# Attention scores of a chunk in two halves of 64 keys, in a token-mixer kernel

## The chip, the cores and the metric

The kernel runs on one core of a Trainium2 chip. The metric is the time of one execution on the device in microseconds (us), as a median of several executions.

## The reference

Three blocks follow one another: a gated linear attention, and two token and channel mixers. The change touches only the first. Cut to what matters, it is, for 4 batches, 8 heads, 768 tokens and 48 features a head:

```python
def _attn_ref(q, k, v, a_re, a_im):
    ...
    for t in range(S):
        new_re = ar * S_re - ai * S_im
        new_im = ar * S_im + ai * S_re
        kv = np.einsum('bhd,bhe->bhde', k[:, :, t], v[:, :, t])
        S_re, S_im = (new_re + kv, new_im)
        y[:, :, t] = np.einsum('bhd,bhde->bhe', q[:, :, t], S_re)
```

Each output row sees the keys and values of its own and of earlier tokens alone.

## The kernel before, in words

The four batches run one after the other. In each, the 768 tokens are cut into C = 6 chunks of P = 128. The real and imaginary parts of a head's 48 features stand together on 96 partitions (2 * HD), so that a token pair's decayed product is one product over 96 rows.

For a chunk c of a batch, TensorE works in the order written in `attention(b, c)`: `key_columns` (transposes of the chunk's keys), `scores(b, c, 0)` and `scores(b, c, 1)` (four heads each, into one PSUM bank each), `outputs` of the chunk before (transposes), `keys_values` (the chunk's contribution to the running state), `values` (scores times values, plus state times queries, into bank 3), and `turn_state` (transposes). In chunk 5 four `rank` products stand in the place of `keys_values`. A matmul on float32 operands is two passes in the trace, each with a weight load of its own.

The score bank holds, for a head, keys on the partitions and queries along the columns: 128 by 128. `mask_scores` on VectorE multiplies a bank of four heads by the triangle `tri` into `ST`, which `values` then takes as its moving operand. The even heads' results stand on partitions 0 to 47 of bank 3 and the odd heads' on 64 to 111 (`lo = 64 * (h % 2)`); `keys_values` is laid out in the same way.

VectorE's order in a batch is `mask_scores(b, c, 0)`, `mask_scores(b, c, 1)`, then `queries_keys(b, c + 2)` (one `scaled`, line 924, and two `turned`, line 937), then `next_state(b, c)`. The scaled queries and keys of chunk c + 2 go from SBUF to the tile `rows[c % 3]` by four DMAs in `to_rows` (lines 333 and 334), and `scores(b, c + 2)` waits for all four. The DMAs are issued from SyncE's one queue in program order; in a batch that order is `load_qk(b, c + 3)`, `load_v(b, c + 2)`, `to_rows(b, c + 2)`. `values` and `keys_values` wait for the semaphore `s_v_in` of `load_v` (line 317, tiles `v_in`), and `scaled` for that of `load_qk`.

At the start VectorE clears two PSUM banks (lines 1151 and 1152), GpSimd builds `tri` and the identity, ScalarE works on the first loads of a, and VectorE's first step of the real work is line 841. In batch 0 the conversion of the weights (ScalarE line 802, GpSimd line 506) runs between the chunks.

The rest of a batch, some 130 us of it, is made of the two mixers, with TensorE busy nearly throughout.

Of the kernel before, what the change touches and what calls it, by code (L numbers as in the profile page):

```python
# [8 lines left out]
ALU = mybir.AluOpType  # L9
ACT = mybir.ActivationFunctionType  # L10

P = 128
CONSTANTS = 6
# [13 lines left out]
        return b * (self.per_batch * self.unit) + (n + self.ahead) * self.unit  # L27


def token_mixer_program(nc, v, qk_rows, a_rows, U, V, w1, w2, w_tc, w_tok, out):  # L30
    B, S, D = v.shape
    HD = 48
    H = D // HD
    PAIRS = H // 2
    C = S // P
# [4 lines left out]
    N2 = HALF * P  # L40
    PIECES = C
    MID = P // 2
    G = D // P
    WIDE, FINE = 2 * HD // G, HD // G
    assert FINE * H == P and 2 * WIDE * H // 2 == 2 * P and C == 2 * G and G == 3
    assert N2 == D and H * HD == D and 3 * R <= P and F * P == 2 * C * P and F == 2 * C
    assert 2 * D == C * P

    with ExitStack() as ctx:
        def sb(name, shape, dt=F32):  # L50
            return ctx.enter_context(nc.sbuf_tensor(name, shape, dt))

        def sem(name, per_batch, unit=1, ahead=0):
            return Count(ctx.enter_context(nc.semaphore(name)), per_batch, unit, ahead)
# [11 lines left out]
        tc_raw = nc.alloc_sbuf_tensor_at("tc_raw", [P, 2 * KD, D], F32, offset=tc_at + 2 * KD * D * 4)  # L66
        U3 = sb("U3", [P, C, 3, R])
        V3 = sb("V3", [3 * R, S], F32R)
        tri = sb("tri", [P, P])
        ident = sb("ident", [P, P])  # L70
        half_pi = sb("half_pi", [P, 1])
        ln_eps = sb("ln_eps", [P, 1])
# [1 line left out]

        marks = sb("marks", [P, 2, G, C])
        minus_mid = sb("minus_mid", [P, G, C])
        gain = sb("gain", [P, G, C - 1])
        gain_rows = sb("gain_rows", [P, H, C - 1])
        carry = sb("carry", [P, G])

# [7 lines left out]
        stream = sb("stream", [P, 4 * 2 * S])  # L88
# [6 lines left out]
        angle = ((tA, tB), (tC, tD))  # L95
        v_in = (stream[:, 8 * D:9 * D], stream[:, 9 * D:10 * D], tD[:, :])
        KV = tA[:, :].rearrange("p (j d) -> p j d", j=PAIRS)
        scale = sb("scale", [P, 2, G, 2, P])
        qk_at = nc.sbuf_base
        qk = sb("qk", [P, 6 * D])  # L100
# [5 lines left out]
        ST = sb("ST", [P, H, P])  # L106
# [7 lines left out]
        rows = [at.rearrange("p (h j t) -> p h j t", h=H, j=2) for at in rows_at]  # L114
# [63 lines left out]
        score_bank = (bank[6], bank[7])  # L178
# [5 lines left out]
        def heads(ap, n=4):  # L184
            return ap.rearrange("p (h t) -> p h t", h=n)


        s_const = sem("s_const", 0)
        s_zero = sem("s_zero", 0)
# [9 lines left out]
        s_a_first = [sem(f"s_a_first{c}", 0, 16) for c in range(C)]  # L199
        s_a_in = [sem(f"s_a_in{i}", 2 if i + A_BUFS < C else 1, 16) for i in range(A_BUFS)]  # L200
        s_qk_in = [sem(f"s_qk_in{i}", C // 2, 16) for i in range(2)]
        s_v_in = [sem(f"s_v_in{i}", C // 3, 16) for i in range(3)]
        s_rows_in = [sem(f"s_rows_in{i}", C // 3, 64) for i in range(3)]
        s_gain_in = sem("s_gain_in", 1, 64)
        s_sq = sem("s_sq", C)
# [93 lines left out]
        def _(sp):  # L299
# [13 lines left out]
            def load_v(b, c):  # L313

                if c >= 3:
                    sp.wait_ge(s_yt.sem, s_yt.at(b, c - 2))
                sp.dma_start(v_in[c % 3], v[b, c * P:(c + 1) * P, :]).then_inc(s_v_in[c % 3].sem, 16)

            def to_rows(b, c):

                if c >= 3:
                    sp.wait_ge(s_yt.sem, s_yt.at(b, c - 2))
                elif b and c == 2:
                    sp.wait_ge(s_ch.sem, s_ch.at(b - 1, 2 * KD))
                elif b and c == 1:
                    sp.wait_ge(s_mix.sem, s_mix.at(b - 1, 2 * C))
                elif b:
                    sp.wait_ge(s_mix.sem, s_mix.at(b - 1, 2 * C - 2))
                to = rows[c % 3]
                for r in range(2 if b or c else 1):  # L330
                    sp.wait_ge(s_Q.sem, s_Q.at(b, c) + r + 1)
                    wide, fine = row(r)
                    sp.dma_start(to[wide, :, :, :], QKz[c % 2][:, r, 0:2, :, :]).then_inc(s_rows_in[c % 3].sem, 16)  # L333
                    sp.dma_start(to[fine, :, :, :], QKz[c % 2][:, r, 2, :, :]).then_inc(s_rows_in[c % 3].sem, 16)
# [42 lines left out]
            def batch(b, last):  # L377
# [36 lines left out]
                if not last:  # L414
                    sp.wait_ge(s_mix.sem, s_mix.at(b, 2 * C - 3))
                    load_qk(b_next, 0)
                    load_qk(b_next, 1)
                    gains_to_rows(b_next)
                    to_rows(b_next, 0)
                    load_qk(b_next, 2)  # L420
                    sp.wait_ge(s_mix.sem, s_mix.at(b, 2 * C))
                    load_v(b_next, 0)
                    load_v(b_next, 1)
# [139 lines left out]
        def _(act):  # L563
# [92 lines left out]
            def attention(b, c):  # L656
# [6 lines left out]
                if c + 1 < C:  # L663
# [3 lines left out]
                    elif b:  # L667
                        act.wait_ge(s_stored[2].sem, s_stored[2].at(b, 0))
                    a.activation(KV[0:112, :, :], bank[4][0:112, 0:D].rearrange("p (j d) -> p j d", j=PAIRS), ACT.Copy)\
                        .then_inc(s_kv_sb.sem, 1)  # L670
# [165 lines left out]
        def _(dve):  # L836
            d = nc.vector
# [15 lines left out]
            def log_decay(b, c):  # L853
# [11 lines left out]
                if b and i == 0:  # L865
                    dve.wait_ge(s_exp.sem, s_exp.at(b - 1, (half + 1) * G))
                d.tensor_copy(marks[:, :, i, half * G:(half + 1) * G],
                              ln_m2.rearrange("p (t e m) -> p e t m", e=2, m=MID)[:, :, :, MID - 1]).then_inc(s_marks.sem, 1)
                if i == G - 1:
# [75 lines left out]
            def mask_scores(b, c, i):  # L945
                dve.wait_ge(s_score.sem, s_score.at(b, 2 * c + i + 1))
                if c >= 1 and i == 0:
                    dve.wait_ge(s_yt.sem, s_yt.at(b, c))
                elif c == 0 and b:
                    for n in range(2 - i):  # L950
                        dve.wait_ge(s_stored[n].sem, s_stored[n].at(b, 0))
                elif c == 0:
                    dve.wait_ge(s_v3.sem, 2)
                d.tensor_tensor(ST[:, 4 * i:4 * i + 4, :], heads(score_bank[i][:, :]),  # L954
                                tri[:, :].unsqueeze(1).broadcast_to([P, 4, P]), ALU.mult)\
                    .then_inc(s_score_sb.sem, 1)

            def next_state(b, c):
# [190 lines left out]


            d.memset(bank[3][:, :], 0.0).then_inc(s_zero.sem, 1)
            d.memset(bank[4][:, :], 0.0).then_inc(s_zero.sem, 1)

            for c in range(C + 2):
# [22 lines left out]
        def _(pe):  # L1177
            t = nc.tensor

            def mm(o, lhsT, rhs, start=True, stop=True, turned=False):  # L1180
                return t.matmul(o, lhsT, rhs, start=start, stop=stop, is_transpose=turned)  # L1181

            def key_columns(b, c):
                if c >= 1:
                    pe.wait_ge(s_kn.sem, s_kn.at(b, c))
                elif b:
                    pe.wait_ge(s_out.sem, s_out.at(b - 1, 2))
                for r in range(2):
                    pe.wait_ge(s_Q.sem, s_Q.at(b, c) + r + 1)
                    for i in range(G):  # L1190
                        ins = t.transpose(bank[r][:, i * P:(i + 1) * P], QKz[c % 2][:, r, i, 1, :], ident[:, :])  # L1191
                    ins.then_inc(s_ktr.sem, 1)

            def scores(b, c, i):
                pe.wait_ge(s_rows_in[c % 3].sem, s_rows_in[c % 3].at(b, c // 3 + 1))
                if c >= 1:
                    pe.wait_ge(s_score_sb.sem, s_score_sb.at(b, 2 * c - 1 + i))
                for h in range(4):
                    ins = mm(heads(score_bank[i][:, :])[:, h, :], rows[c % 3][0:2 * HD, 4 * i + h, 1, :],
                             rows[c % 3][0:2 * HD, 4 * i + h, 0, :])  # L1200
                ins.then_inc(s_score.sem, 1)

            def keys_values(b, c):
# [12 lines left out]
            def turn_state(b, c):  # L1216
# [3 lines left out]
                for j in range(PAIRS):  # L1220
                    ins = t.transpose(heads(bank[2][0:2 * HD, :])[:, j, 0:112], KV[0:112, j, :], ident[0:112, 0:112])  # L1221
                ins.then_inc(s_kv_t.sem, 1)

            def values(b, c):
                pe.wait_ge(s_v_in[c % 3].sem, s_v_in[c % 3].at(b, c // 3 + 1))
                if c >= 1:
                    pe.wait_ge(s_yt_sb.sem, s_yt_sb.at(b, c))
                    pe.wait_ge(s_state.sem, s_state.at(b, c))
                elif b:
                    pe.wait_ge(s_out.sem, s_out.at(b, 0))  # L1230
                for h in range(H):
                    if h % 4 == 0:
                        pe.wait_ge(s_score_sb.sem, s_score_sb.at(b, 2 * c + h // 4 + 1))
                    lo = 64 * (h % 2)
                    o = heads(bank[3][lo:lo + HD, :])[:, h // 2, :]
                    ins = mm(o, v_in[c % 3][:, h * HD:(h + 1) * HD], ST[:, h, :], stop=c == 0)
                    if c >= 1:
                        ins = mm(o, state[0:2 * HD, h, :], rows[c % 3][0:2 * HD, h, 0, :], start=False)
                ins.then_inc(s_yt.sem, 1)
# [207 lines left out]
                        key_columns(b_next, 0)  # L1447

            pe.wait_ge(s_const.sem, CONSTANTS)
            pe.wait_ge(s_zero.sem, 2)  # L1450
            key_columns(0, 0)
            for b in range(B - 1):
                batch(b, False)
# [50 lines left out]
```

## Time and profile before

| | |
|---|---|
| median of 3 executions | 779.67 us (779.47 to 780.95) |
| profiled execution | 780.54 us, of which the span is 778.8 us |
| TensorE busy (matmul) | 710.3 us, 91% |
| VectorE busy | 503.9 us, 65% |
| ScalarE busy | 417.3 us, 54% |
| mean granted TensorE clock | 0.991 |

The profile shows one execution. The span is from its first to its last instruction. PE is TensorE's matmuls, PEld its weight loads, DVE is VectorE, ACT ScalarE, POOL GpSimd and SPq the queue of SyncE, which issues DMAs. Starts in the timeline and in the chain of waits are in us from the span's start. A name such as `bank<-region` is output from input.

### The profile page before, as it was taken

The numbers are of one execution on the slowest core, as the hardware profiler recorded it, in microseconds if no ns is written. First come the engines' busy times: TensorE is split into PE (matmuls) and PEld (weight loads), VectorE is DVE, ScalarE is ACT, GpSimd is POOL, SyncE is SP. The second block draws the span as 40 slices with busy tenths as digits, with TensorE's granted clock in tenths as the row PEclk, the third lists the DMA queues.
The fourth block names the chain that finished last, engine by engine and source line by source line (L and its number), as shares of the span: only waits on it lengthen the run. The fifth ranks groups of instructions, "written<-read, shape, count | busy, mean of one in ns | idle before, by whom it ended". The sixth has DMA issues, their size and how long they took to land.

```text
span 778.8 us, 13125 instructions
## 1 busy us (share of the span) xinstructions
PE 710.3 (91%) x4944; PEld 683.4 (88%) x4944; DVE 503.9 (65%) x918; ACT 417.3 (54%) x913; POOL 220.8 (28%) x175
## 2 busy tenths in 40 slices
PE   0028999999999999999999999999999999999998
PEld 0027879999999979999999979999999879999998
DVE  6978858699458758597458747597448832224634
ACT  8875757665464636673464637674463621223531
POOL 0003582433430053222530053223440000113350
PEclk9998999999999999999999999999999999999999
DMA  9645540010246850010136950010136840000121
GB/s 325 201 110 144 146 176 5 1 42 1 61 120 192 218 203 21 1 42 0 61 104 193 235 203 21 0 42 1 42 103 183 227 144 37 1 1 1 42 61 61
DMA packets 42734, 73.45 MB, mean 94 GB/s; under 512 B 8784, under 2 KB 23376, under 8 KB 42672
## 3 DMA queue, kind: packets, MB, share of 16 engines
q1 hardware_dynamic: 42384, 72.23, 31.6%
q8 instruction: 39, 0.64, 0.4%
q10 hardware_dynamic: 288, 0.39, 0.2%
q14 instruction: 23, 0.19, 0.1%
HBM read 48.96 MB, written 4.72 MB: 69 GB/s over the span
## 4 chain that ended last, share of the span: by engine, by line
PE 83%; DVE 7%; ACT 4%; DMA 3%; issue 2%; SPq 1%; DVEq 0%; ACTq 0%
PE bank L1181 80%; DMA region<-qk 2%; PE bank L1351 1%; DVE stream L924 1%; PE bank L1262 1%; PE bank L1191 1%; PE bank L1221 1%; DMA region<-stream 1%; DVE logr L862 1%; DVE ST L954 1%; DVE qk L937 1%; DVE phasor L913 0%; DVE phasor L904 0%; SPq L333 0%; ACT scale L626 0%
## 5 line engine op out<-in xcount | busy, mean ns | idle before, releaser
L1181 PE MATMUL bank<-uT,w_sb 128*128 128x384 f32 x864 | 167.8, 342 | 0.0
L1181 PE MATMUL bank<-hT,w_sb 128*128 128x384 f32 x864 | 165.0, 337 | 0.0
L1181 PE MATMUL bank<-tok,z 128*128 128x384 f32 x864 | 158.7, 337 | 0.6 <-issue 0.2
L1181 PEld LDWEIGHTS bank<-uT,w_sb 128*128 128x128 f32 x864 | 153.1, 192 | 1.5 <-ACT uT L691 1.2
L1181 PEld LDWEIGHTS bank<-hT,w_sb 128*128 128x128 f32 x864 | 151.2, 188 | 0.3 <-DVE hT L1083 0.3
L1181 PEld LDWEIGHTS bank<-tok,z 128*128 128x128 f32 x864 | 149.3, 188 | 1.8 <-POOL tok L511 1.8
L1083 DVE SCALAR_TENSOR_TENSOR hT<-bank,hT 128x384 fp32r<-128x384 f32 x96 | 52.8, 550 | 72.0 <-ACT hT L683 71.7
L683 ACT ACTIVATE hT<-bank 128x384 fp32r<-128x384 f32 x96 | 46.5, 484 | 83.3 <-PE bank L1181 83.1
L511 POOL TENSOR_TENSOR tok<-tok_low,tok 128x768 fp32r<-128x768 f32 x20 | 38.1, 1907 | 86.8 <-ACT tok L713 86.8
L1191 PE MATMUL bank<-ident,stream 128*128 128x128 f32 x72 | 11.3, 297 | 48.6 <-DVE stream L937 48.6
L519 POOL TENSOR_TENSOR x_sb<-uT 128x384 f32<-128x384 f32 x24 | 25.1, 1074 | 102.2 <-DVE uT L1077 69.2
L1191 PEld LDWEIGHTS bank<-ident,stream 128*128 128x128 f32 x72 | 9.1, 154 | 49.0 <-issue 48.6
L506 POOL TENSOR_TENSOR w_sb<-w_raw,w_sb 128x768 fp32r<-128x768 f32 x12 | 23.8, 1999 | 75.9 <-ACT w_sb L802 75.9
L525 POOL TENSOR_TENSOR xs<-x_sb,xs 128x384 fp32r<-128x384 f32 x24 | 27.7, 1170 | 54.5 <-ACT xs L700 54.5
L488 POOL TENSOR_TENSOR logr<-stream 128x384 f32<-128x384 f32 x18 | 14.9, 826 | 95.8 <-DMA stream<-in_a 95.7
L1181 PE MATMUL bank<-tc_sb,xs 128*128 128x384 f32 x216 | 41.4, 336 | 0.0
L493 POOL TENSOR_TENSOR phasor<-stream,phasor 128x384 f32<-128x384 f32 x18 | 19.1, 1062 | 74.4 <-ACT phasor L599 74.4
L954 DVE TENSOR_TENSOR ST<-bank,tri 128x512 f32<-128x512 f32 x48 | 32.4, 686 | 11.2 <-PE bank L1181 11.0
L1181 PE MATMUL bank<-region 96*128 96x128 f32 x256 | 33.4, 286 | 6.6 <-DMA region<-stream 4.8
L1181 PE MATMUL bank<-xs,tc_sb 128*128 128x384 f32 x216 | 38.9, 338 | 0.0
L1181 PEld LDWEIGHTS bank<-region 96*128 96x128 f32 x256 | 31.7, 201 | 7.7 <-DMA region<-stream 5.2
L1181 PEld LDWEIGHTS bank<-tc_sb,xs 128*128 128x128 f32 x216 | 37.9, 188 | 0.0
(147 smaller groups left out, 1310.7 us busy)
## 6 DMA issues: line engine op xcount, KB each, us to landing
stream<-in_qk SPq DMA_DIRECT2D x24, 384.0 KB, 3.8
tok_low<-in_w_tok SPq DMA_DIRECT2D x20, 384.0 KB, 3.5
stream<-in_a SPq DMA_DIRECT2D x19, 384.0 KB, 4.4
scale<-in_w_tok SPq DMA_DIRECT2D x16, 384.0 KB, 4.2
w_raw<-in_w SPq DMA_DIRECT2D x12, 384.0 KB, 7.6
region<-qk SPq DMA_DIRECT2D x16, 256.0 KB, 3.6
region<-stream SPq DMA_DIRECT2D x15, 256.0 KB, 3.1
stream<-in_v SPq DMA_DIRECT2D x16, 192.0 KB, 4.9
```

Of the source, the lines that this page charges most:

```text
L488: ins = g.tensor_tensor(to, part, part, ALU.mult)
L493: g.tensor_tensor(phasor[:, c, 1, :], a_part(b, c, 1), phasor[:, c, 1, :], ALU.mult)\
L506: g.tensor_tensor(part[1], raw, part[0].bitcast(F32), ALU.subtract).then_inc(s_split.sem, 1)
L511: g.tensor_tensor(tok[:, m % 4, 1, :], tok_raw(m)[1], tok[:, m % 4, 0, :].bitcast(F32), ALU.subtract)\
L519: g.tensor_tensor(x_sb[:, n, :], uT[:, 0, kd, :].bitcast(F32), uT[:, 1, kd, :].bitcast(F32), ALU.add)\
L525: g.tensor_tensor(xs[0][:, 1, n % KD, :], x_sb[:, n, :], xs[0][:, 0, n % KD, :].bitcast(F32), ALU.subtract)\
L683: a.activation(hT[:, n % 3, 0, :], hidden_bank[n % 3][:, 0:N2], ACT.Relu).then_inc(s_hid_hi.sem, 1)
L862: ins = d.tensor_tensor_scan(ln_m2[:, cols], ln_m2[:, cols], cor[:, cols], 0.0, ALU.add, ALU.subtract)
L954: d.tensor_tensor(ST[:, 4 * i:4 * i + 4, :], heads(score_bank[i][:, :]), tri[:, :].unsqueeze(1).broadcast_to([P, 4, P]), ALU.mult)\
L1083: d.scalar_tensor_tensor(hT[:, n % 3, 1, :], hidden_bank[n % 3][:, 0:N2], 0.0, hT[:, n % 3, 0, :].bitcast(F32), ALU.max, ALU.subtract)\
L1181: return t.matmul(o, lhsT, rhs, start=start, stop=stop, is_transpose=turned)
L1191: ins = t.transpose(bank[r][:, i * P:(i + 1) * P], QKz[c % 2][:, r, i, 1, :], ident[:, :])
```

## The change

The scores of a head are no longer one matmul of 128 keys by 128 queries but two: the first 64 keys with all 128 queries, and the last 64 keys with the last 64 queries. What is left uncomputed is the quarter that the triangle sets to zero. For an even head the first keys stand on partitions 0 to 63 of the bank; for an odd head the halves are exchanged. `mask_scores` therefore multiplies by `both_tri`, the triangle and the triangle with its halves exchanged. The values of the odd heads are needed in the same exchanged order of tokens, and come from DRAM a second time, as an array prepared on the host, by a load of [128, 192] for each chunk. The score banks are cleared once at the start.

```diff
+        both_tri = sb("both_tri", [P, 2, P])
+        tri = both_tri[:, 0, :]
+        v_turned_sb = sb("v_turned_sb", [P, 2, PAIRS * HD])
...
                 sp.dma_start(v_in[c % 3], v[b, c * P:(c + 1) * P, :]).then_inc(s_v_in[c % 3].sem, 16)
+                sp.dma_start(v_odd[c % 3], v_turned[b, c * P:(c + 1) * P, :]).then_inc(s_v_in[c % 3].sem, 16)
...
-                d.tensor_tensor(ST[:, 4 * i:4 * i + 4, :], heads(score_bank[i][:, :]),
-                                tri[:, :].unsqueeze(1).broadcast_to([P, 4, P]), ALU.mult)\
+                d.tensor_tensor(ST[:, 4 * i:4 * i + 4, :].rearrange("p (j e) t -> p j e t", e=2),
+                                score_bank[i][:, :].rearrange("p (j e t) -> p j e t", e=2, t=P),
+                                both_tri[:, :, :].unsqueeze(1).broadcast_to([P, 2, 2, P]), ALU.mult)\
...
             d.memset(bank[3][:, :], 0.0).then_inc(s_zero.sem, 1)
+            for i in range(2):
+                d.memset(score_bank[i][:, :], 0.0).then_inc(s_zero.sem, 1)
+            dve.wait_ge(s_const.sem, CONSTANTS)
+            d.tensor_copy(both_tri[0:MID, 1, :], tri[MID:P, :])
+            d.tensor_copy(both_tri[MID:P, 1, :], tri[0:MID, :]).then_inc(s_tri.sem, 1)
+            dve.wait_ge(s_tri.sem, 1)
             d.memset(bank[4][:, :], 0.0).then_inc(s_zero.sem, 1)
...
-                for h in range(4):
-                    ins = mm(heads(score_bank[i][:, :])[:, h, :], rows[c % 3][0:2 * HD, 4 * i + h, 1, :],
-                             rows[c % 3][0:2 * HD, 4 * i + h, 0, :])
+                for pair in range(2):
+                    for late in range(2):
+                        for odd in range(2):
+                            h, lo, t0 = 2 * pair + odd, MID * (odd ^ late), MID * late
+                            ins = mm(heads(score_bank[i][lo:lo + MID, :])[:, h, t0:P],
+                                     rows[c % 3][0:2 * HD, 4 * i + h, 1, t0:t0 + MID],
+                                     rows[c % 3][0:2 * HD, 4 * i + h, 0, t0:P])
...
-                    ins = mm(o, v_in[c % 3][:, h * HD:(h + 1) * HD], ST[:, h, :], stop=c == 0)
+                    of = v_odd[c % 3][:, h // 2 * HD:(h // 2 + 1) * HD] if h % 2 else v_in[c % 3][:, h * HD:(h + 1) * HD]
+                    ins = mm(o, of, ST[:, h, :], stop=c == 0)
```

## Rows read from the trace of the kernel before

**Rows 1.** The page: busy time of the engines, and the shares of the chain that ended last.

```profile
PE 710.3 (91%) x4944; PEld 683.4 (88%) x4944; DVE 503.9 (65%) x918; ACT 417.3 (54%) x913; POOL 220.8 (28%) x175
...
PE 83%; DVE 7%; ACT 4%; DMA 3%; issue 2%; SPq 1%; DVEq 0%; ACTq 0%
```

**Rows 2.** Groups by form, TensorE: busy us, mean ns of one, idle before (scores, values, keys_values).

```profile
L1181 PE MATMUL bank<-region 96*128 96x128 f32 x256 | 33.4, 286 | 6.6 <-DMA region<-stream 4.8 <-DMA region<-qk 1.7
L1181 PE MATMUL bank<-ST,stream 128*48 128x128 f32 x256 | 26.5, 292 | 3.9 <-DVE ST L954 3.8
...
L1181 PE MATMUL bank<-qk,stream 128*48 128x96 f32 x256 | 14.5, 258 | 0.3
```

**Rows 3.** Timeline of TensorE, batch 1, chunk 1 and the start of chunk 2: start, duration.

```profile
250.52 0.87 PE L1181 MATMUL bank<-qk,stream 128*48 128x96 f32 x16
251.22 0.42 PE L1181 MATMUL bank<-ST,stream 128*48 128x128 f32 x4
...
252.75 0.42 PE L1181 MATMUL bank<-stream,state 96*48 96x128 f32 x4
253.11 0.59 PE L1221 MATMUL bank<-ident,tA 112*96 112x112 f32 x4
253.53 0.82 PE L1191 MATMUL bank<-ident,stream 128*128 128x128 f32 x6
254.19 1.95 PE L1181 MATMUL bank<-region 96*128 96x128 f32 x16
```

**Rows 4.** The chain that ended last, batch 1, chunks 0 to 3: start, duration, what.

```profile
246.22 0.96 DVE stream L924
...
251.27 0.96 DVE stream L924
...
255.19 5.42 DMA region<-qk
260.62 0.04 issue
260.66 2.05 PE bank L1181 x16
```

**Rows 5.** The same chain in batches 2 and 3, the last DMA before chunk 3.

```profile
431.97 5.21 DMA region<-qk
...
610.02 6.40 DMA region<-qk
```

**Rows 6.** Timeline of batch 1: a load of values, and two waits for a DMA.

```profile
251.93 0.43 SPq L317 DMA_DIRECT2D stream<-in_v  x1
...
257.37 0.96 DVE L924 TENSOR_TENSOR stream<-stream,scale 128x768 f32<-128x768 f32 x1 [0.50 <-DMA stream<-in_qk]
...
260.66 1.60 PE L1181 MATMUL bank<-region 96*128 96x128 f32 x12 [0.36 <-DMA region<-qk]
```

**Rows 7.** DMA issues of the page: count, size, median us from issue to landing.

```profile
stream<-in_qk SPq DMA_DIRECT2D x24, 384.0 KB, 3.8
...
stream<-in_v SPq DMA_DIRECT2D x16, 192.0 KB, 4.9
```

**Rows 8.** Stretch of 4 us in batch 1: busy time of each engine, clock, DMA share, GB/s.

```profile
256.00:260.00 4.00, 4.00 (x63) 3.67 (x62) 3.29 (x4) 2.46 (x7) 0.00 (x0) 1.00 1.09 277
```

**Rows 9.** Timeline of batch 0, chunks 0 and 1.

```profile
55.06 3.78 PE L1181 MATMUL bank<-region 96*128 96x128 f32 x16 [4.77 <-DMA region<-stream]
...
58.77 1.52 PE L1181 MATMUL bank<-qk,stream 128*48 128x96 f32 x16
...
61.91 0.59 PE L1221 MATMUL bank<-ident,tA 112*96 112x112 f32 x4
...
69.92 0.67 PE L1181 MATMUL bank<-ST,stream 128*48 128x128 f32 x4 [3.63 <-DVE ST L954]
```

**Rows 10.** A stretch of batch 0: busy time of each engine, granted clock (0.51), DMA.

```profile
68.60:72.00 3.40, 2.08 (x20) 2.09 (x22) 3.35 (x5) 2.31 (x3) 0.00 (x0) 0.51 0.02 5
```

**Rows 11.** Timeline of VectorE at the start.

```profile
1.52 0.48 DVE L1152 MEMSET bank<- 128x512 f32 x1
...
4.96 0.56 DVE L841 SCALAR_TENSOR_TENSOR logr<-logr,phasor 128x384 f32<-128x384 f32 x1 [2.95 <-ACT phasor L583]
```

More of the change, by code:

```diff
@@ L27, in at, with token_mixer_program @@
         return b * (self.per_batch * self.unit) + (n + self.ahead) * self.unit
-def token_mixer_program(nc, v, qk_rows, a_rows, U, V, w1, w2, w_tc, w_tok, out):
+def token_mixer_program(nc, v, v_turned, qk_rows, a_rows, U, V, w1, w2, w_tc, w_tok, out):
     B, S, D = v.shape
@@ L42, in token_mixer_program @@
     MID = P // 2
+    ZEROED = 4
     G = D // P
@@ L68, in token_mixer_program @@
         V3 = sb("V3", [3 * R, S], F32R)
-        tri = sb("tri", [P, P])
+        both_tri = sb("both_tri", [P, 2, P])
+        tri = both_tri[:, 0, :]
+        v_turned_sb = sb("v_turned_sb", [P, 2, PAIRS * HD])
         ident = sb("ident", [P, P])
@@ L97, in token_mixer_program @@
         KV = tA[:, :].rearrange("p (j d) -> p j d", j=PAIRS)
+        v_odd = (stream[:, 10 * D + 2 * H * P:10 * D + 2 * H * P + PAIRS * HD], v_turned_sb[:, 0, :], v_turned_sb[:, 1, :])
         scale = sb("scale", [P, 2, G, 2, P])
@@ L201, in token_mixer_program @@
         s_qk_in = [sem(f"s_qk_in{i}", C // 2, 16) for i in range(2)]
-        s_v_in = [sem(f"s_v_in{i}", C // 3, 16) for i in range(3)]
+        s_v_in = [sem(f"s_v_in{i}", C // 3, 32) for i in range(3)]
+        s_tri = sem("s_tri", 0)
         s_rows_in = [sem(f"s_rows_in{i}", C // 3, 64) for i in range(3)]
@@ L1449, in _ @@
             pe.wait_ge(s_const.sem, CONSTANTS)
-            pe.wait_ge(s_zero.sem, 2)
+            pe.wait_ge(s_zero.sem, ZEROED)
             key_columns(0, 0)
@@ L1472, in features_first, with odd_heads_halves_turned @@
         return np.concatenate([wide, rest], axis=1)
+    def odd_heads_halves_turned(x):
+        b, h, s, d = x.shape
+        odd = x.transpose(0, 2, 1, 3)[:, :, 1::2, :].reshape(b, s // P, 2, P // 2, -1)
+        return np.ascontiguousarray(odd[:, :, ::-1]).reshape(b, s, -1)
     def shape(x):
         return x.shape[0], x.shape[2], -1
-    arrays = {"v": tokens_first(inputs["v"])}
+    arrays = {"v": tokens_first(inputs["v"]), "v_turned": odd_heads_halves_turned(inputs["v"])}
     qk = np.stack([features_first(inputs[n]) for n in ("q", "k")], axis=3)
```

## The prediction

> **What bounds the kernel now.** I read the page first: TensorE is busy for 91% of the span and the chain that ended last runs through it for 83% [rows 1]. That would say that whatever TensorE is spared is won, but the share is a mean over stages, and the change lies in the attention stage alone. So I read the groups by form for the matmuls it touches [rows 2], the timeline of a chunk [rows 3], and then the chain through that stage, which decides. In batch 1 the chain is not TensorE's for chunks 0 to 3: it goes from VectorE's scaling of chunk 2's queries and keys at 246.22 to that of chunk 3's at 251.27, then through the issue of four DMAs to the last one's landing, 5.42 us from 255.19, and only then to scores of chunk 3 at 260.66 [rows 4]. Batches 2 and 3 show the same DMA, 5.21 and 6.40 us [rows 5]. TensorE waits 0.36 us there in batch 1 [rows 6]. While these DMAs are under way the DMA share is 1.09, at 277 GB/s [rows 8]: in this stretch the rings are full, and TensorE is close behind them. From chunk 4 on and through the mixers the chain is TensorE's.
>
> **Scores, the matmuls.** A pass over the full width comes every 0.111 us: 16 passes take 1.95 us, of which the last lasts 0.28, so (1.95 - 0.28) / 15 [rows 2, 3]. Values, 48 weight columns on alternating partition halves, starts 32 passes between 251.22 and the end at 253.17: (1.95 - 0.27) / 31 = 0.054 us each, although one pass lasts as long as before [rows 2, 3]. So two column halves of the array run side by side. I take this for the new scores as well: each half then carries, for a pair of heads, two passes over 128 queries (0.111) and two over 64 (half, 0.056, an estimate), 0.334 us; two pairs in a bank 0.67 against 8 x 0.111 = 0.89. That is 0.22 us a bank and 0.44 us a chunk. Bounds: the 64-query passes may cost no less than 0.083, twice keys_values' 0.042 per start ((0.87 - 0.25) / 15 [rows 2, 3]), which leaves 0.22 a chunk; and not less than in proportion, which is what I take.
>
> **Switching between widths.** The last pass of values starts at about 253.17 - 0.27 = 252.90 and turn_state's first at 253.11, 0.21 later, and turn_state takes 0.04 longer than 0.26 + 3 x 0.095 for its four passes [rows 3]. Against the 0.11 of a normal step that is 0.14 us for a switch between full and half width. Now a chunk has two (into keys_values, out of values). With narrow scores between key_columns and outputs, chunks 1 to 5 have two more, +0.28; chunk 0 has no outputs behind its scores, so one switch only moves, and it has none more. Net: -0.44 in chunk 0, -0.16 in chunks 1 to 5.
>
> **The second load of values.** 96 KB for each chunk, issued behind load_v and ahead of to_rows. SyncE pays another 0.43 us for each [rows 6]. Before rows of chunk 3 it has to issue two of them (chunks 2 and 3), which uses up the gap between 252.36 (251.93 + 0.43 [rows 6]) and the issue of 253.28, three DMAs of 0.6 before 255.19 [rows 4]. On the rings: 98304 B at 277 GB/s are 0.355 us each [rows 8]. Bounds: nothing, where a ring has room; and 0.71 if a packet of 768 B costs what one of 1536 B does, which is the load of v, 192 KB, at the same rate [rows 7, 8]. The traffic of this stretch goes by bytes as far as the rows tell, so I take 0.355. Ahead of chunk 4's rows stand three such loads: +1.07 us; the queue of work starts 0.3 us earlier (the second mask of chunk 0 follows scores, 0.44 - 0.14 for the switch in front), so at most +0.77. Where the rings are not all full it is the issue alone that counts, about +0.2, since scaling chunk 4 already waits 0.50 for its load of queries and keys and that load gets later by one of the new ones [rows 6]. I take +0.55 at scores of chunk 4. All that TensorE wins in chunks 0 to 3 is lost in these waits.
>
> **A batch, 1 to 3.** +0.55 until scores of chunk 4. Then chunk 4 gives back 0.44 - 0.14 = 0.30, since its first switch falls into the wait, and chunk 5 gives 0.16. Together +0.09 a batch, +0.3 for three.
>
> **Batch 0.** The rings have room here (0.02 at 68.6 [rows 10]), so the new loads cost nothing. Scores of chunk 0 are on the chain behind the rows' landing, and run at half speed: 3.78 us, a pass every (3.78 - 0.4) / 15 = 0.225 [rows 9]. In the new form 0.67 x 2 x 0.225 / 0.111 = 2.71 instead of 16 x 0.225 = 3.60, -0.89, and the switch into keys_values (58.77) is gone, another -0.2. But turn_state at 61.91 runs at full speed now [rows 9]; if the clock rises when it does now, its four passes come before that and cost about 0.45 more. So -0.65 at VectorE's state. Values of chunk 1 wait for VectorE at 69.92 [rows 9] and follow it. They and the transposes run until 75.5 at a granted clock of 0.51 [rows 10], that is at 1.2 of 2.4 GHz, after TensorE had idled for 3.63 us; with an earlier start more of that work falls in the slow time, +0.3. Chunks 2 and 5 give 0.16 each; chunks 3 and 4 are off the path. Sum -0.65 + 0.3 - 0.32 = -0.7.
>
> **The rest costs nothing.** The mask has the same 512 columns on 128 partitions and should take what it takes. Two memsets of 0.48 us and two small copies end by about 3.7, and VectorE's first real step waits until 4.96 [rows 11]; without that cover they would cost 1.5 us. The values matmuls keep their shape. Clearing happens once.
>
> **Sum.** +0.3 - 0.7 = -0.4 us: 780.1 for the profiled execution (780.54). That one is 0.87 above the median of 779.67, so 779.3 for the median. About 0.2%, or 1.56 us, is what a measurement of this kernel can tell from no change.
>
> **Two rules against the rows.** Values' starts every 0.054 us with four passes of one head before four of the next [rows 3] need passes of the two halves to overtake each other. The Trainium skill ("TensorE: Matmul & The Clock Gate", Part 3, The mechanism) says that matmuls start and end strictly in program order; by that rule eight passes of values would take six steps of 0.111, one every 0.08 us, and the trace does not agree. By its rule the new scores would be slower than the old ones; that is the third rival below. The same page of the Trainium skill (Part 1, on the gap of 56 ns) gives about 62 ns of the sequencer per matmul, by which a chunk's new scores would take 2.0 us. Keys_values shows a start every 0.042 us over 16 passes [rows 3], and the new scores need one every 0.042 over 32; no row shows yet whether that holds for so long.
>
> **Rivals.** *First, faster: the loads find room.* The landing is late by a backlog, not by rate: its 5.42 us compare with a median of 3.8 for a larger load [rows 4, 7]. If the new loads fall in gaps, the rows come 0.3 us earlier with VectorE, and each batch gains 0.3 + 0.30 + 0.16 = 0.76: -2.3 - 0.7 = -3.0, 776.7. If in batch 0 the clock also rises sooner after values' start at 69.3, up to 1.5 more. Against it speaks the DMA share of 1.09.
>
> *Second, slower: the rings decide.* At 0.71 us a load, chunk 4's rows come 3 x 0.71 - 0.3 = 1.8 later, +1.4 a batch, +4.1 - 0.7 = +3.4: 783.1. It decides (slower by over 1.56) from about 0.5 us a load on, at 3 x 0.5 - 0.3 - 0.46 = 0.74 a batch. For it speaks that batch 3 already has a landing of 6.40 [rows 5], against it that bytes seem to rule.
>
> *Third: no overtaking, or issue binds.* With starts in order, a pair's eight passes run 0.111 x 3 + 0.056 x 3 = 0.50 instead of 0.334, against 0.445 before: +0.22 a chunk, with switches +0.5. On the path that is 0.36 (chunk 4) + 0.5 (chunk 5) + 0.7 for the loads, 1.5 a batch, and 1.1 in batch 0: +5.6, 785. If issue keeps no more than the 0.054 us that values show over 32 passes, a chunk's scores take 1.73, nothing is won there either, and the end is near +4. Against it speak the rows of values.
>
> **Chances and range.** Forecast 0.40 (own range 778.2 to 780.6), first rival 0.28, second 0.20, third 0.12. Faster by over 0.2%: nearly all of the first and a little of the forecast, 0.31. Slower: the third and most of the second, 0.27. The rest 0.42. The range reaches below the first rival without the clock's share, 776.2, and up to the second, 783.0; outside are the third and the ends.
>
> **What would show it.** Right: 32 matmul records for a chunk's scores with starts every 0.04 us, a chunk's scores in about 1.6 us with latency; an idle of 0.2 before scores and before outputs; scores of chunk 3 and 4 of batches 1 to 3 still released by the DMA of rows, later against scores of chunk 0 by 0.3 to 1; mask 0.69. Wrong: scores that take 2 us or more (third rival), or a wait for rows that is gone (first), or one grown by over a microsecond (second), or another clock in 50 to 75 us.

## Result and the profile after

The changed kernel takes 787.94 us (median of 4, 784.12 to 789.59) against 779.57 us for the kernel before: the ratio is 1.0102, with a 95% interval of 1.0073 to 1.013. It is slower by 1%, about 8 us, where I had forecast a gain of 0.4. The profiled execution took 787.88 us, its span is 786.1 us, and its mean granted TensorE clock 0.98 instead of 0.991.

The narrow scores themselves did what was expected of them. In the groups by form (columns as in [rows 2]) each pair of passes has become four, half of them over 64 queries:

```profile
L1194 PE MATMUL bank<-region 96*64 96x128 f32 x256 | 25.9, 301 | 12.6 <-DMA region<-qk 7.7 <-DMA region<-stream 4.8
...
L1194 PE MATMUL bank<-region 96*64 96x64 f32 x256 | 19.8, 236 | 0.0
```

The idle time before them is what is new: 7.7 us end in a landing of `region<-qk`, where the kernel before had 1.7 [rows 2]. The timeline of batch 1 of the kernel after shows where (chunks 2 and 3, as [rows 6]):

```profile
250.90 1.29 SPq L323 DMA_DIRECT2D stream<-in_v_turned  x1
...
252.22 1.56 PE L1194 MATMUL bank<-region 96*64 96x128 f32 x32
...
255.57 0.96 DVE L930 TENSOR_TENSOR stream<-stream,scale 128x768 f32<-128x768 f32 x1 [1.05 <-DMA stream<-in_qk]
...
260.17 2.01 PE L1194 MATMUL bank<-region 96*64 96x128 f32 x32 [2.09 <-DMA region<-qk]
```

A chunk's 32 passes of scores take 1.56 us from the first start to the last end, against 1.95 for 16 [rows 3]. TensorE now waits 2.09 us for the rows of chunk 3 instead of 0.36, VectorE 1.05 instead of 0.50 for the load of queries and keys [rows 6], and one issue of the new load blocks SyncE for 1.29 us. And scores of chunk 3, behind that wait, take 2.01 us instead of 1.56. In batch 3 the wait is 3.29 us; there the kernel before already waited 1.34 (its timeline of TensorE):

```profile
616.46 2.05 PE L1181 MATMUL bank<-region 96*128 96x128 f32 x16 [1.34 <-DMA region<-qk]
```

The chain that ended last, in batches 1, 2 and 3 of the kernel after (three answers, columns as in [rows 4]):

```profile
254.20 5.93 DMA region<-qk
...
260.17 2.01 PE bank L1194 x32
...
433.01 5.86 DMA region<-qk
...
438.92 2.83 PE bank L1194 x32
...
442.69 3.94 PE bank L1194 x48
...
447.80 1.49 PE bank L1194 x32
...
449.82 2.60 PE bank L1194 x48
...
614.23 7.41 DMA region<-qk
...
621.68 1.73 PE bank L1194 x32
```

The last DMA ahead of chunk 3 takes 5.93, 5.86 and 7.41 us, against 5.42, 5.21 and 6.40 [rows 4, 5]. In batch 2 the scores behind it take 2.83 us on the chain, and values and keys_values 3.94, where those of chunk 4 take 1.49 and 2.60. The stretches of 4 us around that wait tell why (columns as in [rows 8], the number before the DMA share is the granted clock):

```profile
436.00:440.00 4.00, 1.72 (x18) 1.48 (x18) 2.85 (x4) 3.03 (x11) 0.00 (x0) 0.82 1.07 331
440.00:444.00 4.00, 4.00 (x46) 3.60 (x44) 2.85 (x4) 0.49 (x1) 0.00 (x0) 0.50 1.07 220
444.00:448.00 4.00, 4.00 (x48) 3.64 (x47) 2.00 (x4) 1.58 (x4) 0.00 (x0) 0.82 0.79 203
```

TensorE idled 2.28 us before 438.92, and its granted clock was 1.2 instead of 2.4 GHz from 438.6 to 445.4. In batches 1 and 3 it was 1.2 GHz from 261.1 to 264.5 and from 622.9 to 626.3. In the kernel before, the attention of batches 1 to 3 has no half clock at all.

**Where the 7.3 us of span went.** I take the starts of scores of each chunk from the timelines of TensorE. From scores of chunk 0 to scores of chunk 5 the kernel before needs 28.54, 28.39 and 29.65 us in batches 1, 2 and 3, the kernel after 30.63, 32.12 and 31.63: +2.1, +3.7 and +2.0. In batch 0 it needs 37.14 instead of 38.62: -1.5. The mixers between are the same to 0.3 us, except the last batch's tail, 151.9 instead of 150.7. Both executions have a stretch of half clock in batch 2's mixers (from 461.2 before, from 465.9 after); the one after has another in the tail (from 646.8). That this one comes from the change isn't shown: the profile of the run without the second load, below, has one there too (from about 635.5). The mixers' three stretches give -0.4 in sum, the start up to the first scores +0.2 (55.23 against 55.06), and -1.5 + 7.8 + 1.2 - 0.4 + 0.2 are the 7.3.

Within a batch, two things add up. First, chunk 3 starts later counted from chunk 0's scores: 18.16, 18.17 and 19.15 us against 17.04, 16.81 and 18.01, so +1.1, +1.4 and +1.1. Of this the issue of the last DMA of rows makes 0.6, 0.7 and 0.1 (12.19, 12.26 and 11.70 us after chunk 0's scores, against 11.57 in all three), and its landing 0.5, 0.65 and 1.0. Second, from chunk 3 to chunk 4 it is 7.34, 8.81 and 7.34 us, against 6.12, 6.20 and 6.25 in the kernel before: +1.2, +2.6 and +1.1. At full clock and without waiting the narrow form of this work takes 5.79, which the run with a filler below shows, so the half clock makes 1.6, 3.0 and 1.6 of it. From chunk 4 to chunk 5 the kernel after wins 0.25 a batch (5.14 against 5.38).

### The profile page after: what moved, and what is told of

Same layout as the page of the kernel before. It is cut to its first block, busy times and chain, and to the rows that moved or that the text cites. A ratio compares the mean times of both kernels' runs of the same rounds, so it can differ in the third digit from the quotient of the medians.

```text
span 786.1 us, 13921 instructions
## 1 busy us (share of the span) xinstructions
PE 710.4 (90%) x5328; PEld 679.4 (86%) x5328; DVE 504.9 (64%) x922; ACT 416.6 (53%) x913; POOL 221.4 (28%) x175
## 4 chain that ended last, share of the span: by engine, by line
PE 84%; DVE 5%; ACT 4%; DMA 3%; SPq 2%; issue 2%; ACTq 0%; DVEq 0%
PE bank L1194 80%; DMA region<-qk 2%; PE bank L1280 1%; PE bank L1369 1%; PE bank L1204 1%; PE bank L1238 1%; DMA region<-stream 1%; SPq L339 1%; DVE logr L868 1%; DVE phasor L910 0%; ACT scale L632 0%; SPq L340 0%; DMA stream<-in_a 0%; DVE Z L1071 0%; DVE stream L930 0%
## 5 line engine op out<-in xcount | busy, mean ns | idle before, releaser
L1194 PEld LDWEIGHTS bank<-region 96*64 96x64 f32 x512 | 25.7, 150 | 16.0 <-DMA region<-qk 8.4
L1194 PE MATMUL bank<-region 96*64 96x128 f32 (+1 forms) x512 | 28.1, 269 | 12.6 <-DMA region<-qk 7.7
L960 DVE TENSOR_TENSOR ST<-bank,both_tri 128x512 f32<-128x512 f32 x48 | 31.7, 684 | 12.1 <-PE bank L1194 12.0
```

What stands on the lines that cost most here:

```text
L960: d.tensor_tensor(ST[:, 4 * i:4 * i + 4, :].rearrange("p (j e) t -> p j e t", e=2), score_bank[i][:, :].rearrange("p (j e t) -> p j e t", ...
```

## The experiments

Each kernel was timed in five rounds against the kernel before on the same chip. The times of the kernel before were 779.46, 779.41 and 780.89 us in the three groups of runs, so I go by the ratios.

### The changed kernel without the second load

```diff
-                sp.dma_start(v_odd[c % 3], v_turned[b, c * P:(c + 1) * P, :]).then_inc(s_v_in[c % 3].sem, 16)
...
-                    of = v_odd[c % 3][:, h // 2 * HD:(h // 2 + 1) * HD] if h % 2 else v_in[c % 3][:, h * HD:(h + 1) * HD]
+                    of = v_in[c % 3][:, h * HD:(h + 1) * HD]
```

> Scores stay in halves; the second load of values is taken out, and odd heads take the first load's values in unexchanged order (so their outputs are other numbers). Theory R (the second load delays the rows of chunk 3 in batches 1 to 3, TensorE idles over 2 us there and its clock falls to half): the wait before scores of chunk 3 is below 1.2 us, no half clock in the attention of batches 1 to 3, time 775 to 778 us. Theory N (the half-width matmuls themselves leave TensorE idle or throttled): waits of 2 us and more stay, 784 us or more.

Measured: 776.64 us, ratio 0.9956 (0.9938 to 0.9974). This is theory R's case: the half-width scores with all their switches are worth 0.4%, and the load costs all of that and 1% more. The wait before chunk 3, expected below 1.2 us, is 1.25 in batch 1, 0.16 in batch 2 and nothing in batch 3; before chunk 4 TensorE waits 0.96, 1.61 and 1.03 us. Here is the one in batch 1 (timeline of TensorE):

```profile
258.39 1.56 PE L1193 MATMUL bank<-region 96*64 96x128 f32 x32 [1.25 <-DMA region<-qk]
```

So even without the new load the faster scores run into the rows' DMAs at chunks 3 and 4, and a part of their gain is lost there. In this execution none of these waits brought a half clock in the attention of batches 1 to 3; scores take 1.56 us behind each.

### The kernel before with the second load

The edit adds the load, its array, its tiles and its count on the semaphore `s_v_in` to the kernel before; nothing reads what it brings.

```diff
                 sp.dma_start(v_in[c % 3], v[b, c * P:(c + 1) * P, :]).then_inc(s_v_in[c % 3].sem, 16)
+                sp.dma_start(v_odd[c % 3], v_turned[b, c * P:(c + 1) * P, :]).then_inc(s_v_in[c % 3].sem, 16)
```

> The kernel before with the second load of values added, not used by anything. Theory R: the wait before scores of chunk 3 grows from 0.3 to 1.5 by 0.7 to 1.5 us, with half clock in one or more batches where it passes 2 us: 782 to 786 us. Theory N: the load is hidden, within 1.5 us of the kernel before.

Measured: 784.9 us, ratio 1.0066 (1.0042 to 1.0089). The load alone costs 0.7%, without any narrow score. In its profile batch 1 waits 1.12 us before chunk 3, where the kernel before waited 0.36; batch 3 waits 1.22, no more than the 1.34 of the kernel before; and batch 2 waits at chunks 2 and 4 instead:

```profile
432.60 2.05 PE L1184 MATMUL bank<-region 96*128 96x128 f32 x16 [0.80 <-DMA region<-stream]
...
445.46 1.72 PE L1184 MATMUL bank<-stream 96*128 96x128 f32 x13 [0.71 <-DMA stream<-stream]
```

I had expected half clocks too; the profiled execution, 782.7 us and the second fastest of six, has none in the attention of batches 1 to 3. The direction and size are theory R's, the step through the clock isn't shown by this one. A longer wait before chunk 3 it shows in batch 1 alone.

Without load and with it, the wide scores give 1 and 1.0066, the narrow ones 0.9956 and 1.0102. So the load costs 0.7% beside wide scores and 1.5% beside narrow ones. The two parts of the change work against each other in the kernel after: narrow scores bring TensorE to the rows earlier, the load makes the rows later, both stretch one wait, and behind that wait the clock fell.

### A filler in the place of the wait

```diff
+    FILL = 9
...
             def scores(b, c, i):
+                if b and c == G and i == 0:
+                    pe.wait_ge(s_score_sb.sem, s_score_sb.at(b, 2 * c - 1 + i))
+                    for _ in range(FILL):
+                        mm(score_bank[0][:, 0:P], ident[:, :], ident[:, :])
```

> The changed kernel; in batches 1 to 3, nine full-width matmuls on the identity (18 passes, 2.0 us) stand ahead of TensorE's wait for the rows of chunk 3, results overwritten. If the half clock after the wait is what idling brings, it is gone, scores of chunk 3 to chunk 5 take 12 us instead of 12.5 to 14, and the time is 782 to 785 us, 3 to 6 below the changed kernel's 788. If the fall of the clock has another cause, or costs nothing, the time stays at 787 to 790.

Measured: 782.02 us, ratio 1.0031 (1.0017 to 1.0045). Fifty-four passes of useless work, 2.17 us three times, make the changed kernel faster by 0.7%. In batch 2 of its profile they stand ahead of chunk 3, whose scores then take 1.56 us; but chunk 4 waits 1.78 us there, and behind that wait the half clock is back, with 2.83:

```profile
434.69 2.17 PE L1195 MATMUL bank<-ident 128*128 128x128 f32 x18
436.79 1.56 PE L1195 MATMUL bank<-region 96*64 96x128 f32 x32
444.44 2.83 PE L1195 MATMUL bank<-stream 96*64 96x128 f32 x32 [1.78 <-DMA stream<-stream]
```

In batch 3 the same work from chunk 3 to chunk 4 takes 5.79 us (620.06 to 625.85), the full-clock value used above. Scores of chunk 3 to those of chunk 5 take 11.70, 15.98 and 10.92 us, so the expected 12 failed in batch 2. The fall of the clock after the wait is therefore what costs at least about half of the load's 1.5%.

The same filler in the version below, whose waits at chunk 3 are short, is the control:

> The version with the second load moved out of the stage, plus the same filler as before ahead of the rows of chunk 3. Its waits there are 0.3 to 0.8 us and its clock does not fall, so if the filler helped the changed kernel through the clock alone, it costs here: 2.0 us of passes less a wait of 0.2 to 0.8, up to 3 x 1.5, partly taken out of chunk 4's wait: 777 to 781 us, not below 776.8. If the filler helps in some other way (as by warming the array for narrow matmuls), the time falls below 776.

Measured: 777.71 us, ratio 0.9973 (0.9959 to 0.9987), against 0.9960 (0.9945 to 0.9975) without the filler. It does not help here, where the profile without it has no half clock in the attention of batches 1 to 3, and seems to cost 0.1%, though the intervals overlap. Its profile has no wait for rows at all in batches 1 to 3, and a whole stretch of 7.80 us from chunk 2 to chunk 3 in each.

**The clock in all executions.** Every execution is recorded with its span and mean granted clock. Span times (1 - clock) is the time that TensorE lost to half clock as recorded, and at most what that added to the span, since half clock costs nothing while TensorE idles. Means over each kernel's executions, in us:

| | time | lost to half clock | the rest |
|---|---|---|---|
| kernel before (24 executions) | 779.5 | 5.8 | 773.7 |
| kernel before with the second load (6) | 784.7 | 7.6 | 777.1 |
| changed, without the second load (7) | 776.1 | 5.9 | 770.3 |
| changed (4) | 787.4 | 13.6 | 773.9 |
| changed, with filler (12) | 782.0 | 7.5 | 774.4 |

The second load adds 3.3 us of rest beside wide scores and 3.6 beside narrow ones, nearly the same. What makes it dearer beside narrow scores is the clock, +1.8 against +7.7 us, and the filler takes 6.0 of that away. So up to two thirds of what the load costs the changed kernel is half clock, and the changed kernel differs from the kernel before in that column alone: the rest is level (773.9 and 773.7), as narrow scores take from it what the load adds.

### Issue without bytes, and half the bytes

```diff
-                sp.dma_start(v_odd[c % 3], v_turned[b, c * P:(c + 1) * P, :]).then_inc(s_v_in[c % 3].sem, 16)
+                sp.dma_start(v_odd[c % 3][0:1, :], v_turned[b, c * P:c * P + 1, :]).then_inc(s_v_in[c % 3].sem, 16)
```

> As without the second load (odd heads take the first load's values, so their outputs are other numbers), but SyncE still issues a DMA in its place, of one packet of 768 B instead of 128. Theory R, rings: as without the load, 775 to 778. Theory I (what costs is SyncE's time to issue, 0.43 us a DMA ahead of the rows): 1 to 3 us above the run without load, wait before chunk 3 grown by 0.3 to 0.9; if it is all of the cause, 785 or more.

Measured: 778.98 us, ratio 0.9989 (0.9965 to 1.0012), single times from 772.34 to 781.78. The median lies 2.3 us over the run without load, as theory I's smaller case says, but the intervals of the two ratios overlap and the profiled execution is the fastest of all (772.34). I leave it at that: the issue costs somewhere between nothing and 0.6%, and not the whole.

```diff
+                sp.dma_start(v_odd[c % 3][:, 0:2 * HD], v_turned[b, c * P:(c + 1) * P, 0:2 * HD]).then_inc(s_v_in[c % 3].sem, 16)
```

> The changed kernel, but the second load brings only the first 96 of its 192 columns: the same 128 packets at 384 B, the same issue, half the bytes (heads 5 and 7 take other heads' values, so their outputs are other numbers). Between 776.6 without load and 788 with it: if bytes on the rings count, 780 to 784; if packets or the issue count, 786 to 789.

Measured: 781.91 us, ratio 1.0025 (1.001 to 1.004), half way between 0.9956 and 1.0102. With packets and issue unchanged, halving the bytes takes away 0.8% of the 1.5%. It scatters as the others do, from 778.13 to 787.82, and the profiled execution is the slowest; in batch 3 it waits 2.19 us before chunk 3.

### The load behind the rows

The second loads of chunks 3 to 5 are issued behind the rows of the same chunk; those of chunks 0 to 2 stay where they were.

```diff
                     if c + 2 < C:
                         to_rows(b, c + 2)
+                    if c >= 1 and c + 2 < C:
+                        load_v_odd(b, c + 2)
```

> The changed kernel with the second load of chunks 3 to 5 issued behind the rows of the same chunk instead of ahead of them; same bytes in the stage. If its place in the queue ahead of the rows is what counts, the wait before chunk 3 shrinks by 0.5 to 1 us, mostly without half clock: 781 to 785 us. If only the sum of bytes in the stage counts, chunk 4 pays instead: 786 to 789.

Measured: 783.61 us, ratio 1.0047 (1.0022 to 1.0072), single times from 777.29 to 787.68. The place in the queue counts for about a third of the load's cost, with wide intervals; the rest stays, as the bytes stay in the stage. In its profile batch 2 still idles long enough before chunk 3 to start it 8.29 us after chunk 2, batch 3 only 5.86. The wait in batch 2 is longer than that of the kernel after in batches 1 and 2, and no half clock follows it:

```profile
440.14 1.56 PE L1201 MATMUL bank<-region 96*64 96x128 f32 x32 [2.43 <-DMA region<-qk]
```

In batch 1 of the same profile a wait of only 1.45 us is followed by half clock from 261.6 to 265.0. So the length of the wait alone doesn't say whether the clock falls.

### The load out of the stage

The tile of exchanged values gets four slots; chunks 0 to 3 come by one DMA of 384 KB during the mixers of the batch before, chunk 4 at their end, chunk 5 behind the rows of chunk 5.

```diff
+            def load_v_odd(b, part):
+                if part == 0:
+                    src = v_turned[b, 0:4 * P, :].rearrange("(c p) d -> p c d", p=P)
+                    sp.dma_start(v_turned_sb[:, :, :], src).then_inc(s_v_odd[0].sem, 16)
+                else:
+                    c = 3 + part
+                    if c == C - 1:
+                        sp.wait_ge(s_yt.sem, s_yt.at(b, 1))
+                    sp.dma_start(v_odd[c], v_turned[b, c * P:(c + 1) * P, :]).then_inc(s_v_odd[part].sem, 16)
...
                 load_tok(b, 1)
+                if not last:
+                    load_v_odd(b_next, 0)
```

> The changed kernel with the second load out of the crowded stage: chunks 0 to 3 in one DMA during the mixers before, chunk 4 at the end of the mixers, chunk 5 behind the rows of chunk 5. Theory R (rings and queue between chunks 1 and 4): as without the load, 775 to 779 us, below the kernel before's 779.5; waits at chunks 3 and 4 of 0.5 to 1.8 us as there. If the values' reads or the load at large cost, 784 or more.

Measured: 776.82 us, ratio 0.9960 (0.9945 to 0.9975). It leaves nothing out of the computation, is faster than both kernels, and is level with the run without any second load: with four of a batch's six loads moved to the mixers before and the fifth to their end, the same bytes cost nothing that can be measured. In batch 2 of its profile chunks 2, 3 and 4 start so:

```profile
428.39 1.56 PE L1212 MATMUL bank<-region 96*64 96x128 f32 x32
434.78 1.56 PE L1212 MATMUL bank<-region 96*64 96x128 f32 x32 [0.53 <-DMA region<-qk]
440.79 1.56 PE L1212 MATMUL bank<-stream 96*64 96x128 f32 x32 [0.15 <-DMA stream<-stream]
```

To see whether the rings limit even this version, two stores of 192 KB of the batch before, which stand ahead of chunk 4's rows, were put behind chunk 5's:

```diff
-                    if b and c == 1:
+                    if b and c == 3:
                         store(b - 1, KD)
```

> The version with the second load moved out, and the two stores of 192 KB of the batch before, now issued ahead of chunk 4's rows, put behind chunk 5's. If the rings are what chunks 3 and 4 still wait for (0.4 to 1.0 us each there), the wait before chunk 4 falls by 0.3 to 1 us a batch: 774 to 776.3 us. If it is VectorE's order or the issue, no change from 776.8.

Measured: 776.81 us, ratio 0.9951 (0.9932 to 0.9971). That is not to be told from 0.9960. In the profiled execution chunk 4 no longer waits in any batch, as the rings would have it, but chunk 3 does, up to 2.3 us, with a half clock behind it in batch 1. Whether the move of the stores or the scatter between executions puts the waits there stays open.

## Why the prediction was wrong

**Scores, the matmuls: right.** For a chunk 32 starts at 0.042 us were taken, 1.34 in all; at full clock the last pass starts 1.34 us after the first. Passes of the two halves overlap and overtake as values' do, 32 passes at 0.042 us do not outrun the issue, and the third rival fell. On the two rules weighed in the prediction, from the Trainium skill ("TensorE: Matmul & The Clock Gate", Part 3, The mechanism, and Part 1): the trace of after agrees neither with starts and ends strictly in program order nor with 62 ns of sequencer for each matmul. For the 62 ns the Trainium skill names a condition, hardware decoding switched off, that the prediction left out and that no run here shows.

**Switching: nearly right.** In the timeline outputs of chunk 0 start 1.49 us after the start of scores of chunk 1, and a chunk without waits takes 5.79 us instead of 5.94: -0.15, where -0.16 was taken.

**Batch 0: right in direction, about half the size.** -0.7 was taken, -1.5 came in the attention. Counted from chunk 0's scores, VectorE's `state_sum` starts 1.25 us earlier (61.45 instead of 62.53), where -0.65 was taken; the 0.45 for a turn_state at half speed did not come, as the one at 60.39 took 0.59 us. Scores of chunk 2 start 1.6 earlier; from there to chunk 5 it is 0.1 more, where -0.32 was taken for chunks 2 and 5. Why that gain stayed out was not followed up.

**The start: right.** The two memsets (1.03 us), two copies of 0.22 and the last memset end at 3.70, and the first step starts at 5.19 with 1.48 us of idle before it.

**The second load: this is the step that failed.** "I take +0.55 at scores of chunk 4" was the term; what came is +2.3, +4.0 and +2.2 (chunk 4's scores counted from chunk 0's: 25.50, 26.98 and 26.49 us against 23.16, 23.01 and 24.26). Two errors lie in it. The smaller is the landing: chunk 3 came 1.1 to 1.4 later, where by the same working two loads less the head start give +0.4. The issue was taken at 0.43 for each load, but an issue took up to 1.29 us in this stage. The larger was left out altogether. I had written that what TensorE wins in chunks 0 to 3 "is lost in these waits", and had in the same text a row where TensorE idles 3.63 us and then runs at 0.51 of its clock [rows 9, 10], and did not put the two together: a faster TensorE and a later landing add up to one idle of over 2 us, and work behind it runs at half speed. That is 1.6, 3.0 and 1.6 us. The filler shows it by taking most of it away. The wait itself was read in batch 1 alone, 0.36 us; in batch 3 it stood at 1.34 already.

The second rival, "the rings decide", had place and direction right, at 783.1 us, and nearly the size of the delay: for chunk 3 its working gives 2 x 0.71 - 0.3 = +1.1, and +1.1, +1.4 and +1.1 came. But 0.6, 0.7 and 0.1 of that are the later issue and not the rings, the run with half the bytes speaks against its reason that packets rather than bytes count, and this rival had no half clock behind the delay either. The first rival was wrong for this kernel: the loads found no room where they were put. That the run with the load moved comes to 776.82, next to its 776.7, does not bear out its reason.

What stays open: how much of the landing's delay is the issue and how much the rings. The run with one packet and the run behind the rows bound it (0 to 0.6% and about 0.5% of 1.5%), but their scatter of 9 to 10 us between executions of the same kernel is larger than what is to be told apart. The recorded clocks show what the scatter goes with. The fastest and slowest executions of the run behind the rows, 777.29 and 787.68 us, have mean clocks of 0.996 and 0.983, which is 10.3 us of half clock more in the slow one; of the run with one packet, 772.34 and 781.78 us have 0.996 and 0.987, or 7.0 us. What decides whether the clock falls behind a given wait stays open.

## What to carry to other kernels

Before TensorE's work is made shorter in a stage, read what ends its waits there: where a DMA does, the gain turns into idle time, and idle time may be paid for twice, in waiting and in a half clock behind it. A change that spares TensorE and adds a transfer in the same stage is to be priced as one thing, not as the sum of its two parts: here -0.4% and +0.7% gave +1.0%. Put the added transfer where the rings are idle, even if it takes more SBUF; the same bytes cost 1.5% in the crowded stage (0.9956 to 1.0102) and nothing measurable when most of them came during the mixers before (0.9960).

## What was not expected of the hardware

- In the kernel after, each wait for the rows of chunk 3 (2.09, 2.28 and 3.29 us) was followed by TensorE at half clock, for 3.4, 6.8 and 3.4 us. In other runs waits of 1.45 us (load behind the rows, batch 1) and 1.78 us (filler, batch 2) were followed by it too, and waits of 1.61 us (without load, batch 2) and 2.43 us (load behind the rows, batch 2) were not.
- Eighteen passes on a constant, 2.17 us, ahead of such a wait are worth more than they cost (1.0102 to 1.0031).
- The issue of one DMA on SyncE's queue took 1.29 us (0.43 before) while the DMA share of the stage was 1.00 over 18 us (0.94 before); another, of rows, took 1.10. The run without the second load has one of 1.19 as well (429.62, rows of chunk 3), so they are not the new load's alone.
- From full-width work to half-width work, and from values to turn_state, 0.20 us pass from the start of the last pass to the start of the next weight load, from the 64-query passes to outputs 0.15; and 32 half-width passes of 128 and 64 columns start at 0.042 us on average.
